# Attention and MLP in one kernel: in the first batch the softmax division moves from the probabilities to the output of head pairs

## The chip, the cores and the metric

The kernel runs on one core of one Trainium2 chip. The metric is the device time in microseconds (us) of one execution; every time here is in us unless marked ns. The engines are TensorE (PE in the rows; its weight loads are PEld), VectorE (DVE), ScalarE (ACT), GpSimd (POOL) and SyncE (SP), which issues the DMAs. Each works through its own list of instructions in order, and semaphores make one wait for another.

## What is computed

Three layers in fp32, on 4 batches of 576 tokens with 8 heads of 64:

```python
scores = (q @ k.T) / 8 + (cum_i - cum_j)      # decay; masked above the diagonal
attn = exp(scores - max(scores))
attn = attn / (sum(attn) + 1e-9)              # the division that the change moves
x = attn @ v                                  # per head; heads side by side: 2304 x 512
h = x @ w_in                                  # 512 x 2048
x2 = (h * sigmoid(1.702 * h)) @ w_out         # 2048 x 512
# then a soft mixture of 8 experts over 32 slots, on x2: 2304 x 512 out
```

## The kernel before

**Precision.** Matmul operands are split into a high and a low part (`kh` and `kl`, `pth` and `ptl`, `xh` and `xl`, and so on): ScalarE or VectorE makes the high part by a copy that rounds, VectorE or GpSimd the low part by a subtraction.

**Stages.** `run` (line 374) gives every engine the same sequence of batches. In batch 0 (`begin`) attention runs alone: the MLP has no input yet. From then on the MLP of batch b is laid between the attention steps of batch b + 1, in units. At the end come the last MLP alone and the expert layer.

**Slots.** `batch_steps` (line 88) writes each engine's order out by hand, in slots. Slot s holds the scoring of head s (scores, decay, Exp, sums) and the second half of head s - 1 (transposes of its probabilities, PV, output). The first batch has slots 0 to 8; slot 0 has no second half, and slot 8 scores head 0 of batch 1, while its second half is head 7 of batch 0. What the order lists of the first batch are (lines 148, 150 and 153) can be read in the code below. The steps that the text speaks of:

- `qk` of the head after next's slot: six transposes of q and k on TensorE into bank `xb` (line 924), then ScalarE makes `qs` (587) and `kh` (589), VectorE the low part of q (711) and `kl` (715). `dup`: GpSimd doubles `kh` and `kl` into the other 64 partitions (534, 536), by adding a column of zeros from `mask`, repeated.
- `score` in four groups g = 0 to 3: matmuls into `yb` (944, 946). The query rows of a head stand in five tiles, 0 to 4; group 0 is tile 4 (64 rows, 576 columns), then tile 3 (512), tiles 2 and 0 (384, 128), and tile 1 (256). VectorE adds the decay and takes the minimum (728), ScalarE takes Exp with the sum (595). Group 0 of the next head comes early, at the end of a slot (`early`).
- `vsplit` (VectorE 735, GpSimd 542), then `norm`: VectorE adds 1e-9 to the sums (740), takes the reciprocal (742) into `rsum`, and scales tiles 0 to 3 of `prob` in place (747); ScalarE scales tile 4 (602).
- `pt` in four chunks c = 0 to 3: TensorE transposes the scaled tiles into `zb` (963); ScalarE copies to `pth` (608), VectorE subtracts to `ptl` (753).
- `fill`: 16 matmuls into `mb`, the MLP's banks, whose results nobody reads (969; only in the first batch).
- `pv_first` and `pv`: TensorE multiplies v by `pth` and `ptl` into `xb` (990), with the part of v's high half in partitions 0 to 63 and of its low half in 64 to 127. `pv_first` also waits for `kl` of a later head, because `xb` holds q and k's transposes too. ScalarE copies the lower half to `olow` (613), and VectorE adds both halves into `xst` (759), 64 partitions for an even head and 64 for an odd one, so that a pair of heads fills one tile of `xst`.
- `xsplit`, in slot 8: ScalarE makes `xh` (617), VectorE `xl` (764) from the four tiles of `xst`; TensorE's MLP (1041) starts behind them.
- `weights` and `split`: in a few slots a 128x512 piece of the MLP's weights is loaded and split, by VectorE (705) and GpSimd (571).

Semaphores: `expd` counts Exp tiles, `sum_inv` reciprocals, `normed` and `normed_4` the scalings, `o_sum` the output sums.

Of the kernel before, what the change touches and what calls it, by code (L numbers as in the profile page):

```python
# [28 lines left out]
P = 128  # L29
# [17 lines left out]
S4_AT = 224  # L47
TURNS = [[(0, 0, 0), (0, 1, 0), (0, 2, 0), (0, 3, 0)],
# [39 lines left out]
def batch_steps(engine, begin, heads, following, mlp):  # L88
# [13 lines left out]
    for slot in range(0 if begin else 1, HEADS + 1):  # L102
# [9 lines left out]
        def at(yes, *step):  # L112
            return [(ahead, step)] if yes else []
# [16 lines left out]
        norm = at(scoring, "norm", s)  # L130
        end = at(scoring, "vsplit", s) + norm
        pv_first, pv = at(before, "pv_first", s - 1), at(before, "pv", s - 1)

# [8 lines left out]
        if begin:  # L142

            steps += [(0, ("weights", t)) for t in {1: (0, 1), 4: (2,), 5: (3,), 6: (4,), 7: (5,)}.get(slot, ())]
            steps += [(0, ("split", slot - 3))] if 2 < slot < 7 else []

            if engine == "pe":
                steps += pt(0) + pt(1) + score(1) + score(2) + qk + pt(2) + score(3) + pt(3) + at(before, "fill", s - 1) + pv_first + early + pv
            elif engine == "act":
                steps += (pt(0) + score(0) + pt(1) + score(1) + qk + pt(2) + score(2) + dup + pt(3) + score(3)  # L150
                          + norm + early_x + pv + xs[3])
            else:
                steps += (pt(0) + score(1) + pt(1) + score(2) + qk + pt(2) + score(3) + dup + pt(3)
                          + end + early + early_x + pv + xs[3])
            continue
# [15 lines left out]
def build(nc, q, k, v, f, w_in, w_out, phi, w1, w2, out):  # L171
    ctx = ExitStack()
    with ctx:
# [70 lines left out]
        rsum = sb("rsum", [P, 2, QT], F32, att_mem)  # L244
# [47 lines left out]

        xbf = xb[:, :, :].rearrange("p a n -> p (a n)")
# [38 lines left out]
        normed_4 = sem("normed_4")  # L332
        p_tr = sem("p_tr")
# [180 lines left out]
        def _(pool):  # L514
# [12 lines left out]
            def step(b, m, st):  # L527
# [10 lines left out]
                elif st[0] == "vsplit":  # L538
# [4 lines left out]
                                       vs[:, s % 2, :, 0:DIM].bitcast(F32), ALU.subtract).then_inc(v_split, 1)  # L543
                elif st[0] == "split":
# [34 lines left out]
        def _(act):  # L579
# [3 lines left out]
            def step(b, m, st):  # L583
# [6 lines left out]
                elif st[0] == "score":  # L590
                    s, par = st[1], st[1] % 2
                    for i in SCORE_ORDER[st[2]]:
                        w, r = P * i + QW[i], QW[i]
                        act.wait_ge(decayed, b * 40 + 5 * s + TILE_RANK[i] + 1)
                        nc.scalar.activation(prob[0:r, par, POFF[i]:POFF[i] + w], prob[0:r, par, POFF[i]:POFF[i] + w],  # L595
                                             ACT.Exp, bias=m_row[0:r, par, i:i + 1], scale=-1.0,
                                             accum_out=sums[0:r, par, i:i + 1]).then_inc(expd, 1)
                elif st[0] == "norm":
# [3 lines left out]
                    nc.scalar.activation(t, t, ACT.Copy, scale=rsum[0:QW[4], par, 4:5]).then_inc(normed_4, 1)  # L602
# [11 lines left out]
                elif st[0] == "xsplit":  # L614
                    kt = st[1]
                    act.wait_ge(o_sum, m * 8 + 2 * kt + 2)
# [63 lines left out]
        def _(dve):  # L680
# [26 lines left out]
            def step(b, m, st):  # L707
# [28 lines left out]
                elif st[0] == "norm":  # L736
# [5 lines left out]
                    nc.vector.reciprocal(rsum[:, par, :], sums_e[:, par, :]).then_inc(sum_inv, 1)  # L742
                    dve.wait_ge(sum_inv, n + 1)
                    for i in range(QT - 1):
                        w, r = P * i + QW[i], QW[i]
                        t = prob[0:r, par, POFF[i]:POFF[i] + w]
                        ins = nc.vector.tensor_scalar(t, t, rsum[0:r, par, i:i + 1], None, ALU.mult)  # L747
# [7 lines left out]
                elif st[0] == "pv":  # L755
# [4 lines left out]
                                            olow[r0:r0 + 64, :], ALU.add).then_inc(o_sum, 1)  # L760
                elif st[0] == "xsplit":
# [147 lines left out]
        def _(pe):  # L909
# [5 lines left out]
            def step(b, m, st):  # L915
# [241 lines left out]
```

## Time and profile before

| | |
|---|---|
| median of 3 runs | 823.66 us (822.15 to 827.57) |
| profiled execution | 823.54 us, of which the span in the trace 821.7 |
| busy, share of the span | PE 91%, PEld 85%, DVE 65%, ACT 46%, POOL 46% |
| first batch alone (attention without MLP) | about 9 to 107 us |
| chain of waits over the whole span, by engine | PE 64%, DVE 16%, issue 8%, ACT 4%, DMA 4% |

A share of busy time is an average over stages. The first batch, about an eighth of the span, is the only stretch in which the changed steps run, and there the engines stand otherwise than over the whole: it has to be read by itself. "Idle before" with an arrow names what ended a wait.

### The profile page before, as it was taken

Reading aid. Unit: us, or ns where it says so; the run is one execution under the profiler, and the core shown is the slowest. Engines: PE = TensorE matmul, PEld = TensorE weight load, DVE = VectorE, ACT = ScalarE, POOL = GpSimd, SP = SyncE. Lnnn points to the kernel's source line nnn. Section 1 sums busy time; section 2 is a strip of 40 time slices with the busy share of each in tenths; the row PEclk is TensorE's granted clock in tenths of the full one; section 3 lists DMA queues with packets and bytes.
Section 4 is the critical chain, followed back from the end, with each engine's and each line's share of the span. In section 5 each row is a group of like instructions: output and inputs, shape, how many; then the busy total and the mean of one; then the engine's idle time right before and its main releaser. Section 6 shows DMA issues by size and latency. Waiting matters only on the chain.

```text
span 821.7 us, 16948 instructions
## 1 busy us (share of the span) xinstructions
PE 751.1 (91%) x5993; PEld 698.9 (85%) x5993; DVE 534.7 (65%) x1430; ACT 374.5 (46%) x903; POOL 376.8 (46%) x394
## 2 busy tenths in 40 slices
PE   3899978999999699999999989999998999996996
PEld 2788878998999689999999889999998999993552
DVE  5899966777677676777777577777675444434323
ACT  3677754545454554546364454545443222111113
POOL 2344335565655165656474164747460776620000
PEclk9999989999999999999999699999999999997995
DMA  4433313333333113333334013333320545497976
GB/s 97 99 85 103 98 33 86 90 90 84 89 98 107 39 53 82 88 95 88 88 88 117 17 45 88 88 89 93 96 65 26 167 148 194 136 346 277 402 307 230
DMA packets 96518, 96.77 MB, mean 118 GB/s; under 512 B 61296, under 2 KB 61296, under 8 KB 96432
## 3 DMA queue, kind: packets, MB, share of 16 engines
q1 hardware_dynamic: 96432, 95.66, 38.5%
q8 instruction: 50, 0.82, 0.4%
q14 instruction: 36, 0.29, 0.1%
HBM read 90.84 MB, written 4.79 MB: 116 GB/s over the span
## 4 chain that ended last, share of the span: by engine, by line
PE 64%; DVE 16%; issue 8%; ACT 4%; DMA 4%; POOL 2%; SPq 1%; DVEq 0%; ACTq 0%; POOLq 0%
PE mb L1041 43%; PE yb L944 4%; PE zb L963 4%; PE xb L990 4%; DVE prob L747 3%; DMA qk_in<-in_k 2%; DVE ptl L753 2%; DMA ring_b<-in_moe_w 2%; PE mb L1016 2%; DVE qs L711 2%; ACT prob L595 1%; DVE kl L715 1%; PE xb L924 1%; PE mb L1080 1%; PE zb L1136 1%
## 5 line engine op out<-in xcount | busy, mean ns | idle before, releaser
L1041 PE MATMUL mb<-xh,wih 128*128 128x288 f32 x512 | 163.5, 319 | 11.4 <-DVE hid L813 7.0
L1041 PE MATMUL mb<-gh,woh 128*128 128x288 f32 x512 | 157.5, 308 | 3.8 <-DVE hid L813 3.8
L1041 PE MATMUL mb<-xl,wih 128*128 128x288 f32 x512 | 155.3, 303 | 0.0
L1041 PE MATMUL mb<-xh,wil 128*128 128x288 f32 x512 | 155.0, 303 | 0.0
L1041 PE MATMUL mb<-gl,woh 128*128 128x288 f32 x512 | 151.0, 295 | 0.0
L1041 PE MATMUL mb<-gh,wol 128*128 128x288 f32 x512 | 151.0, 295 | 0.0
L554 POOL TENSOR_TENSOR gl<-hid,gh 128x288 fp32r<-128x288 f32 x128 | 113.1, 890 | 57.1 <-ACT gh L636 55.8
L571 POOL TENSOR_TENSOR wol<-stage,woh 128x512 fp32r<-128x512 f32 x64 | 82.5, 1288 | 120.0 <-DVE woh L705 120.0
L813 DVE SCALAR_TENSOR_TENSOR hid<-gate,mb 128x288 f32<-128x288 f32 x128 | 57.6, 452 | 103.4 <-ACT gate L642 101.8
L595 ACT ACTIVATE prob<-prob,m_row 64x576 f32<-64x576 f32 (+4 forms) x160 | 96.4, 604 | 59.4 <-DVE m_row L728 58.8
L571 POOL TENSOR_TENSOR wil<-stage,wih 128x512 fp32r<-128x512 f32 x64 | 82.6, 1291 | 81.9 <-DVE wih L705 81.9
L1041 PEld LDWEIGHTS mb<-xh,wih 128*128 128x128 f32 x512 | 100.5, 196 | 13.2 <-DVE hid L813 8.1
L642 ACT ACTIVATE gate<-mb 128x288 f32<-128x288 f32 x128 | 52.7, 411 | 110.6 <-PE mb L1041 110.0
L608 ACT CAST pth<-zb 128x512 fp32r<-128x512 f32 (+1 forms) x128 | 62.9, 492 | 87.5 <-PE zb L963 83.7
L1041 PEld LDWEIGHTS mb<-xl,wih 128*128 128x128 f32 x512 | 100.8, 197 | 0.0
L1041 PEld LDWEIGHTS mb<-xh,wil 128*128 128x128 f32 x512 | 100.5, 196 | 0.0
L1041 PEld LDWEIGHTS mb<-gh,woh 128*128 128x128 f32 x512 | 96.7, 189 | 4.4 <-issue 2.8
L1041 PEld LDWEIGHTS mb<-gl,woh 128*128 128x128 f32 x512 | 96.6, 189 | 0.0
L1041 PEld LDWEIGHTS mb<-gh,wol 128*128 128x128 f32 x512 | 96.3, 188 | 0.0
L728 DVE CUSTOM_DVE_ANT_0 prob<-yb,cum_b 64x576 f32<-64x576 f32 (+4 forms) x160 | 83.5, 537 | 3.2 <-issue 3.0
L963 PE MATMUL zb<-ident,prob 128*128 128x128 f32 x480 | 76.1, 283 | 7.1 <-DVE prob L747 4.4
L753 DVE TENSOR_TENSOR ptl<-zb,pth 128x512 fp32r<-128x512 f32 (+1 forms) x128 | 72.9, 569 | 14.5 <-ACT pth L608 14.2
(145 smaller groups left out, 1450.3 us busy)
## 6 DMA issues: line engine op xcount, KB each, us to landing
stage<-in_moe_w_in SPq DMA_DIRECT2D x64, 256.0 KB, 3.3
stage<-in_moe_w_out SPq DMA_DIRECT2D x64, 256.0 KB, 2.7
ring_a<-in_moe_w SPq DMA_DIRECT2D x16, 1024.0 KB, 7.5
ring_b<-in_moe_w SPq DMA_DIRECT2D x14, 1024.0 KB, 11.6
cum_b<-cum_dram SPq DMA_DIRECT2D x32, 288.0 KB, 4.1
qk_in<-in_q SPq DMA_DIRECT2D x32, 144.0 KB, 3.3
qk_in<-in_k SPq DMA_DIRECT2D x32, 144.0 KB, 3.7
v_in<-in_v SPq DMA_DIRECT2D x32, 128.0 KB, 3.3
```

The source lines that it names most:

```text
L554: pool.tensor_tensor(gl[:, i % FT, HALF * (i // FT):HALF * (i // FT + 1)], hid[:, i % RING, :], gh[:, i % FT, HALF * (i // FT):HALF * (i / ...
L571: pool.tensor_tensor(lo[:, t, :], stage[:, t % 2, :], hi[:, t, :].bitcast(F32), ALU.subtract).then_inc(w_lo, 1)
L595: nc.scalar.activation(prob[0:r, par, POFF[i]:POFF[i] + w], prob[0:r, par, POFF[i]:POFF[i] + w], ACT.Exp, bias=m_row[0:r, par, i:i + 1], s ...
L608: nc.scalar.copy(pth[:, lo:hi], zb[:, c % 2, 0:hi - lo]).then_inc(p_hi, 1)
L642: nc.scalar.activation(gate[:, j % RING, :], mb[:, u % 2, 0:HALF], ACT.Tanh, scale=GATE / 2).then_inc(h_tanh, 1)
L728: nc.vector.tensor_tensor_reduce(prob[0:r, par, o:o + w], ybf[0:r, base:base + w], cum_b[0:r, par, 0:w], 1.0, 3e38, ALU.add, ALU.min, m_ro ...
L753: nc.vector.tensor_tensor(ptl[:, lo:hi], zb[:, c % 2, 0:hi - lo], pth[:, lo:hi].bitcast(F32), ALU.subtract).then_inc(p_lo, 1)
L813: nc.vector.scalar_tensor_tensor(out=hid[:, j % RING, :], in0=gate[:, j % RING, :], scalar=1.0, in1=bank[:, 0:HALF], op0=ALU.add, op1=ALU. ...
L944: mm(ybf[0:r, base + k0:base + k0 + kw], qs[:, par, P * i:P * i + r], x[:, par, k0:k0 + kw], start=not last, stop=last, skip_group_check=True)
L963: ins = tr(zb[:, c % 2, at:at + P], prob[:, par, POFF[i] + P * kt:POFF[i] + P * kt + P], swapped if back else ident)
L990: ins = mm(pv_ps[:, lo:q1], vs[:, par, kt, :], x[:, at:at + q1 - lo], start=(kt == 0 and x is pth), stop=(kt == (1 if q1 == 256 else 4) an ...
L1041: ins = mm(bank[:, 0:HALF], a[:, t, P * (j % 4):P * (j % 4) + P], x[:, t, cols], start=(i == 0), stop=(i == 11))
```

## The change

In the first batch, for heads 0 to 7, the probabilities are no longer scaled. `norm` becomes `sums`, which ends with the reciprocals; TensorE's transposes wait for the last Exp (`expd`) in place of the scaling. From batch 1 on `norm` is as before. In place of the scalings, for each pair of heads:

- `widen`, GpSimd, once a head, behind `vsplit`: writes each row's reciprocal 64 times side by side into `wide` (5 query tiles x 2 heads x 64), by adding the repeated zero column of `mask`. `wide` lies in `x2t`, which the MLP doesn't use yet.
- `spread`, TensorE, once a pair, in the even slots 2, 4, 6 and 8, between `pt` 1 and the first score group: five transposes of `wide` into the MLP's banks `mb`, so that each of the 128 rows of a pair's output finds its factors along the columns. ScalarE copies the 128x576 result to `spread_sb`, behind Exp of the first score group and ahead of the `qk` copies. `fill` waits for that copy.
- `scale`, VectorE, once a pair, right behind the output sum of the odd head: `xst` times `spread_sb`, 128x576. `xsplit` on ScalarE waits for it in the first batch.

`rsum` gets four rows in place of two.

```diff
@@ batch_steps
+        late_norm = begin and slot < HEADS
+        norm = at(scoring, "sums" if late_norm else "norm", s)
         end = at(scoring, "vsplit", s) + norm
+        if engine == "pool" and late_norm:
+            end = end + at(True, "widen", s)
+        spread = at(begin and before and s % 2 == 0, "spread", s - 1)
         pv_first, pv = at(before, "pv_first", s - 1), at(before, "pv", s - 1)
+        if engine == "dve":
+            pv = pv + at(begin and before and s % 2 == 0, "scale", s - 1)
...
             if engine == "pe":
-                steps += pt(0) + pt(1) + score(1) + score(2) + qk + pt(2) + score(3) + pt(3) + at(before, "fill", s - 1) + pv_first + early + pv
+                steps += pt(0) + pt(1) + spread + score(1) + score(2) + qk + pt(2) + score(3) + pt(3) + at(before, "fill", s - 1) + pv_first + early + pv
             elif engine == "act":
-                steps += (pt(0) + score(0) + pt(1) + score(1) + qk + pt(2) + score(2) + dup + pt(3) + score(3)
+                steps += (pt(0) + score(0) + pt(1) + score(1) + spread + qk + pt(2) + score(2) + dup + pt(3) + score(3)
                           + norm + early_x + pv + xs[3])
@@ GpSimd
+                elif st[0] == "widen":
+                    s = st[1]
+                    pool.wait_ge(sum_inv, s + 1)
+                    wait_from(pool, spread_tr, s // 2)
+                    pool.tensor_tensor(wide[:, :, s % 2, :], rsum[:, s % 4, :].unsqueeze(2).broadcast_to([P, QT, DIM]),
+                                       mask[:, 0:1].unsqueeze(1).broadcast_to([P, QT, DIM]), ALU.add).then_inc(widened, 1)
@@ ScalarE
+                elif st[0] == "spread":
+                    pair = (b * 8 + st[1]) // 2
+                    act.wait_ge(spread_tr, pair + 1)
+                    wait_from(act, x_scaled, pair)
+                    nc.scalar.copy(spread_sb, spread_ps).then_inc(spread_out, 1)
...
                 elif st[0] == "xsplit":
                     kt = st[1]
-                    act.wait_ge(o_sum, m * 8 + 2 * kt + 2)
+                    if isinstance(m, int) and m == 0:
+                        act.wait_ge(x_scaled, kt + 1)
+                    else:
+                        act.wait_ge(o_sum, m * 8 + 2 * kt + 2)
@@ VectorE
-                    nc.vector.reciprocal(rsum[:, par, :], sums_e[:, par, :]).then_inc(sum_inv, 1)
+                    nc.vector.reciprocal(rsum[:, s % 4, :], sums_e[:, par, :]).then_inc(sum_inv, 1)
+                    if st[0] == "sums":
+                        return
...
+                elif st[0] == "scale":
+                    n = b * 8 + st[1]
+                    kt = n // 2
+                    dve.wait_ge(spread_out, kt + 1)
+                    dve.wait_ge(o_sum, n + 1)
+                    nc.vector.tensor_tensor(xst[:, kt, :], xst[:, kt, :], spread_sb, ALU.mult).then_inc(x_scaled, 1)
@@ TensorE
-                    if c == 0:
-                        pe.wait_ge(normed, b * 8 + s + 1)
-                    if c == 1:
-                        pe.wait_ge(normed_4, b * 8 + s + 1)
+                    n = b * 8 + s
+                    if isinstance(n, int) and n < HEADS:
+                        if c == 0:
+                            pe.wait_ge(expd, 5 * n + 5)
+                    elif c == 0:
+                        pe.wait_ge(normed, n + 1 - HEADS)
+                    elif c == 1:
+                        pe.wait_ge(normed_4, n + 1 - HEADS)
...
+                elif st[0] == "spread":
+                    n = b * 8 + st[1]
+                    pe.wait_ge(widened, n + 1)
+                    wait_from(pe, spread_out, n // 2)
+                    for i in range(QT):
+                        ins = tr(spread_ps[:, P * i:P * i + QW[i]], wide[0:QW[i], i, :, :].rearrange("p h d -> p (h d)"),
+                                 ident[0:QW[i], 0:QW[i]])
+                    ins.then_inc(spread_tr, 1)
                 elif st[0] == "fill":
+                    wait_from(pe, spread_out, (b * 8 + st[1] + 1) // 2)
```

## Rows read from the trace of the kernel before

**Rows 1.** Busy by stretch: length, PE, PEld, DVE, ACT, POOL, granted clock, DMA, GB/s.
```profile
40.00:60.00 20.00, 18.64 (x144) 16.62 (x144) 19.13 (x60) 15.62 (x38) 9.45 (x11) 1.00 0.38 88
```

**Rows 2.** Chain of waits, first batch: start, duration, engine, tile, line.
```profile
35.88 0.67 DVE xst L759
...
93.82 0.67 DVE xst L759
```

**Rows 3.** Timeline of one period, VectorE: start, duration, engine, line, operation, shapes, count.
```profile
62.18 0.19 DVE L742 RECIPROCAL rsum<-sums_e 128x5 f32<-128x5 f32 x1
...
62.41 1.54 DVE L747 TENSOR_SCALAR prob<-prob,rsum 128x128 f32<-128x128 f32 x4
...
63.87 0.74 DVE L728 CUSTOM_DVE_ANT_0 prob<-yb,cum_b 64x576 f32<-64x576 f32 x1
...
64.65 0.75 DVE L759 TENSOR_TENSOR xst<-xb,olow 64x576 f32<-64x576 f32 x1
...
65.43 0.43 DVE L705 CAST wih<-stage 128x512 fp32r<-128x512 f32 x1
...
65.78 0.69 DVE L753 TENSOR_TENSOR ptl<-zb,pth 128x512 fp32r<-128x512 f32 x1
...
66.39 0.69 DVE L728 CUSTOM_DVE_ANT_0 prob<-yb,cum_b 128x512 f32<-128x512 f32 x1
...
67.00 0.69 DVE L753 TENSOR_TENSOR ptl<-zb,pth 128x512 fp32r<-128x512 f32 x1
...
68.50 0.75 DVE L711 SCALAR_TENSOR_TENSOR qs<-xb,qs 64x576 fp32r<-64x576 f32 x1
...
69.28 0.76 DVE L715 TENSOR_TENSOR kl<-xb,kh 64x576 fp32r<-64x576 f32 x1
```

**Rows 4.** Timeline of the same period: GpSimd, TensorE and ScalarE.
```profile
61.98 0.89 POOL L542 TENSOR_TENSOR vs<-v_in,vs 128x320 fp32r<-128x320 f32 x1 [0.27 <-DVE vs L735]
...
63.27 0.28 PE L990 MATMUL xb<-ptl,vs 128*128 128x64 f32 x1
...
63.58 0.64 ACT L613 COPY olow<-xb 64x576 f32<-64x576 f32 x1 [0.40 <-PE xb L990]
...
63.99 0.97 PEld L963 LDWEIGHTS zb<-ident,prob 128*128 128x128 f32 x9 [0.56 <-DVE prob L747]
...
67.11 0.72 ACT L595 ACTIVATE prob<-prob,m_row 128x512 f32<-128x512 f32 x1 [0.60 <-DVE m_row L728]
...
67.83 0.63 ACT L587 ACTIVATE qs<-xb 64x576 fp32r<-64x576 f32 x1
...
68.24 1.98 PE L969 MATMUL mb<-mask_r,ident_r 128*128 128x128 f32 x16
...
70.29 0.36 PE L990 MATMUL xb<-pth,vs 128*128 128x256 f32 x1
...
70.37 1.15 POOL L536 TENSOR_TENSOR kl<-kl,mask 64x576 fp32r<-64x576 f32 x1
...
71.62 0.32 PE L944 MATMUL yb<-kh,qs 128*64 128x288 f32 x1
```

**Rows 5.** Timeline, end of slot 0: VectorE and TensorE.
```profile
22.57 1.73 DVE L747 TENSOR_SCALAR prob<-prob,rsum 128x128 f32<-128x128 f32 x4
...
23.50 0.31 PE L946 MATMUL yb<-mask_r,ident_r 64*64 64x64 f32 x1
...
24.35 0.90 PE L963 MATMUL zb<-ident,prob 128*128 128x128 f32 x3 [0.54 <-DVE prob L747]
```

**Rows 6.** Timeline at the first batch's end, then (last row) busy time by stretch.
```profile
103.10 2.08 DVE L764 TENSOR_TENSOR xl<-xst,xh 128x576 fp32r<-128x576 f32 x3
...
105.21 0.75 DVE L759 TENSOR_TENSOR xst<-xb,olow 64x576 f32<-64x576 f32 x1
...
107.59 0.60 PE L1041 MATMUL mb<-xh,wih 128*128 128x288 f32 x1 [4.31 <-DVE xl L764]
...
107.00:111.00 4.00, 3.41 (x14) 3.40 (x15) 0.45 (x1) 1.08 (x4) 0.00 (x0) 0.50 0.00 0
```

More of the change, by code:

```diff
@@ L47 @@
 S4_AT = 224
+SPREAD_AT = 128
 TURNS = [[(0, 0, 0), (0, 1, 0), (0, 2, 0), (0, 3, 0)],
@@ L129, in batch_steps @@
             qk, dup = qk + dup, []
-        norm = at(scoring, "norm", s)
+        late_norm = begin and slot < HEADS
+        norm = at(scoring, "sums" if late_norm else "norm", s)
         end = at(scoring, "vsplit", s) + norm
+        if engine == "pool" and late_norm:
+            end = end + at(True, "widen", s)
+        spread = at(begin and before and s % 2 == 0, "spread", s - 1)
         pv_first, pv = at(before, "pv_first", s - 1), at(before, "pv", s - 1)
+        if engine == "dve":
+            pv = pv + at(begin and before and s % 2 == 0, "scale", s - 1)
         xs = [at(s == 0 and before, "xsplit", t) for t in range(KM)]
@@ L243, in build @@
         sums_e = sb("sums_e", [P, 2, QT], F32, att_mem)
-        rsum = sb("rsum", [P, 2, QT], F32, att_mem)
+        rsum = sb("rsum", [P, 4, QT], F32, att_mem)
         f_sb = prob[0:BATCH * HEADS, 0, 0:SEQ]
@@ L291, in build @@
         zb = pb("zb")
+        x2_flat = x2t[:, :, :].rearrange("p t n -> p (t n)")
+        wide = x2_flat[:, 0:QT * 2 * DIM].rearrange("p (i h d) -> p i h d", i=QT, h=2)
+        spread_sb = x2t[:, 2, :]
+        spread_ps = mb[:, :, :].rearrange("p a n -> p (a n)")[:, SPREAD_AT:SPREAD_AT + SEQ]
         xbf = xb[:, :, :].rearrange("p a n -> p (a n)")
@@ L332, in build @@
         normed_4 = sem("normed_4")
+        widened = sem("widened")
+        spread_tr = sem("spread_tr")
+        spread_out = sem("spread_out")
+        x_scaled = sem("x_scaled")
         p_tr = sem("p_tr")
@@ L601, in step @@
                     t = prob[0:QW[4], par, POFF[4]:POFF[4] + SEQ]
-                    nc.scalar.activation(t, t, ACT.Copy, scale=rsum[0:QW[4], par, 4:5]).then_inc(normed_4, 1)
+                    nc.scalar.activation(t, t, ACT.Copy, scale=rsum[0:QW[4], st[1] % 4, 4:5]).then_inc(normed_4, 1)
                 elif st[0] == "pt":
@@ L735, in step @@
                     nc.vector.tensor_copy(vs[:, s % 2, :, 0:DIM], v_in[:, s % 2, :, :]).then_inc(v_hi, 1)
-                elif st[0] == "norm":
+                elif st[0] in ("sums", "norm"):
                     s, par = st[1], st[1] % 2
@@ L746, in step @@
                         t = prob[0:r, par, POFF[i]:POFF[i] + w]
-                        ins = nc.vector.tensor_scalar(t, t, rsum[0:r, par, i:i + 1], None, ALU.mult)
+                        ins = nc.vector.tensor_scalar(t, t, rsum[0:r, s % 4, i:i + 1], None, ALU.mult)
                     ins.then_inc(normed, 1)
```

## The prediction

> **What bounds the kernel now.** The change touches only the first batch, so I first asked the busy table by stretch what bounds that part. In [rows 1] VectorE is busy 19.13 of 20 us, TensorE 18.64, ScalarE 15.62, GpSimd 9.45, at a granted clock of 1.00. VectorE looks like the bound, and the change takes work from it. But a busy share doesn't say what the freed time is worth: the next wait does. So I took the chain of waits, where the first batch shows one pattern per head. The sum of a head's output ends its PV product and stands in it at 35.88 for head 0 and at 93.82 for head 6 [rows 2]: six periods, (93.82 - 35.88) / 6 = 9.66 us each. Then the timeline of one period, VectorE first [rows 3], the other engines second [rows 4].
>
> The four scalings of `prob` by `rsum` stand at 62.41 and take 1.54 us; VectorE gets on with the next tile at 63.87, so their slot in its queue is 63.87 - 62.41 = 1.46 us [rows 3]. Behind them wait the decay of tile 4 of the next head (63.87), then the output sum `xst` (64.65), then the next head's first `ptl` (65.78 behind a weight cast). On TensorE the last matmul of PV starts at 63.27 and lasts 0.28; ScalarE copies the low half to `olow` from 63.58 to 64.22 [rows 4]. The sum needs that copy. So it starts at 64.65 now and can't start before about 64.25, whatever VectorE has to do. What is late next after the scalings is PV, only 0.40 us behind them.
>
> And PV hangs on VectorE's own later work. After `xst` come `ptl`, decay, `ptl` (67.00 to 67.69), then TensorE's third score group and the 16 fill matmuls (68.24 to 70.22), and then PV at 70.29; beside it VectorE makes `kl` by 70.04, which PV awaits too [rows 3, 4]. This closes a loop: PV, `olow`, `xst`, `ptl`, decay, `ptl`, score, fill, PV. One turn costs one period, 9.66 us; of it only 0.40 us is the scaling. The reader is to see that VectorE is full, yet the loop runs through it only in part, and that anything put into the loop is paid in full.
>
> **The change part by part.**
>
> (a) *Scalings removed, heads 0 to 7.* 1.46 us of VectorE's queue each, 11.7 us in all, but worth 0.40 us where the loop closes behind it. That is so at the end of the first batch's slots 1 to 7: 7 x 0.40 = 2.8 us gained. ScalarE's scaling of tile 4 (0.78 us, between the last Exp and `olow`) goes as well; ScalarE waits for PV behind it, so nothing. TensorE's first transposes wait for the last Exp in place of the scaling: they start at 63.99, behind an idle time that ends with the scaling [rows 4], and could start at some 63.55, but their product is next used by VectorE behind `xst`, so nothing more.
>
> (b) *Slot 0* has no PV. There the transposes of head 0 wait for the scaling alone: TensorE's early score ends at about 23.65 (last matmul at 23.50) and the transposes start at 24.35 [rows 5]. Gain 0.7 us; bounds 0.54 (the idle time that the row shows) and 0.85.
>
> (c) *The scale of a head pair on VectorE*, 4 times: 128x576, two SBUF inputs. The same form is `xl`: three take 2.08 us, 0.69 each [rows 6]. It also waits for the sum before it, which costs the overlap of some 0.08 that neighbours in the queue have (66.39 + 0.69 ends after the next starts at 67.00 [rows 3]). I take 0.75 us (bounds 0.61 and 0.78). It stands right behind `xst` and ahead of the next `ptl`, in the loop, with nothing beside it that hides it: 4 x 0.75 = 3.0 us lost. The last of them delays the cast of the fourth x tile, which in the seam starts as soon as `xst` is done (105.21 + 0.75, then the cast, `xl`, and TensorE's first MLP matmul at 107.59 [rows 6]).
>
> (d) *The copy of the spread out of PSUM on ScalarE*, 4 times, slots 2, 4, 6 and 8, placed ahead of the q copy. Its price: `olow` (64x576 from PSUM) is 0.64 us [rows 4]; no 128x576 copy from PSUM is in the trace, and columns set the time of the others, so 0.64. In the row, Exp runs 67.11 to 67.83, the q copy 67.83 to 68.46, and VectorE's q step starts at 68.50 [rows 3, 4]: ScalarE goes ahead without a gap and VectorE waits for it. So the q step moves from 68.50 to 69.14 and `kl` ends at 70.68 in place of 70.04. PV then starts after 70.75 in place of 70.29, a delay of about 0.5. But GpSimd's doubling of `kl` starts at 70.37 and lasts 1.15, and TensorE's early score comes right after it at 71.62 [rows 4]; it moves by the whole 0.64. I take 0.62 (bounds: 0.24, if only TensorE's fill, which now also waits for this copy, counted; 0.76, with VectorE's small gap ahead of the q step added). 4 x 0.62 = 2.5 us lost.
>
> (e) *TensorE's spread*, five transposes a pair: nine take 0.97 us to issue [rows 4], so 0.11 each, 0.55 us. It stands ahead of the first score group. That group can begin 0.44 us earlier than now (a), so it comes 0.1 us later; the decay that reads it starts 0.6 us after its `ptl` and still finds it done. Nothing. Its cover is the time from PV's end to that decay; if it goes, 0.55 x 4 = 2.2 us.
>
> (f) *GpSimd's widening*, eight times, 128x640 in halves of 320 columns. The nearest row is the v split, 320 columns, 0.89 us [rows 4]. It comes behind that split (61.98 to 62.87) and behind the reciprocal (62.18 + 0.19 [rows 3]), so it ends at about 63.8; TensorE wants it at about 64.5, after the nine transposes. Next in GpSimd's queue are a weight split, which waits for VectorE until after `xst`, and the doublings of `kh`, behind the copies that follow 67.83, and of `kl` at 70.37: all far off. Nothing, with 0.7 us in hand.
>
> (g) `rsum` with four rows, and the counts of `normed` less 8 from batch 1 on: no time. DMA issues and SyncE's order don't change. Batches 1 to 3 have the same instructions and move as a block.
>
> **Sum.** -0.7 - 2.8 + 3.0 + 2.5 = +2.0 us. The profiled execution took 823.54 us (span 821.7 and 1.84 around it), so 825.5; it lies 0.12 below the median of the three runs, 823.66, so the comparison holds for the median too.
>
> **A rule weighed.** The scalings in [rows 3] take 1.54 us with GpSimd's v split beside their start, 61.98 to 62.87 [rows 4]; VectorE's tensor-tensor operations don't show such a neighbour's cost in these rows. By the terms above the scale of a pair, at about 65, and the widening, until 63.8, don't meet. The Trainium skill ("SBUF — State Buffer", Who interferes with whom) says that a VectorE instruction with two SBUF inputs contends with a GpSimd instruction that reads SBUF, and the later one waits for the whole of the other; the new scale is such an instruction and speaks against this change. By it the sum would be that of the collision below, if the two met.
>
> **The rivals.**
>
> *VectorE stays the bound.* If the work freed were all worth its time: 8 x 1.46 - 4 x 0.75 = 8.7 us gained, 814.8. For it: 19.13 of 20 busy. Against it: `olow` ends 0.4 us ahead of `xst`, in a fixed order. Chance 0.04.
>
> *The copy is hidden.* If ScalarE or the queue behind it had more room than I read, (d) is nothing: 825.5 - 2.5 = 823.0. For it: ScalarE is idle 4.4 of 20 us. Against it: not there. Chance 0.15.
>
> *The seam costs more.* Between PV of head 7 and the first MLP matmul at 107.59 TensorE has little to do, and in the stretch behind it its granted clock is 0.50, the 1.2 GHz level [rows 6]. The gap grows by 0.75 us. If the low level lasts longer for it, up to the whole of that 4 us stretch at half rate again, 2 to 3 us come on top: about 828. Chance 0.13.
>
> *Collision.* Each pair's scale waits for a widening of 0.89: 4 x 0.89 = 3.6, 829.1. Against it: the 1.2 us between them. Chance 0.04.
>
> *The widening is late: slower by more.* Place: TensorE's spread, ahead of the first score group, with the whole queue (scores, q and k transposes, fill, PV) behind it. It decides once a widening takes over 0.89 + 0.7 = 1.6 us; from there each us costs four. With both operands repeated by a stride of zero, it is unlike the row; at four times its 0.89, 3.6 us, it would be 4 x 2.0 = 8.0, together 833.5. For it: no row has this form. Against it: the doubling of k in [rows 4] also adds a repeated zero column, 576 columns in 1.15. Chance 0.06.
>
> That the change does nothing isn't a case: the scalings are gone from the code.
>
> **How the numbers follow.** The forecast, the loop with (c) and (d) paid, has 0.58. Its bounds are 823.4 (0.24 for the copy and 0.61 for the scale) and 826.2. The runs scatter from 822.15 to 827.57. From the hidden copy less that scatter, to the collision, 821.5 to 829.5 leaves out the first rival and the last, one in ten. 1% is 8.2 us, about what a measurement tells from no change: only the first rival is faster by that (0.04), only the last slower (0.06 with its upper part, 0.05 taken), the rest is within: 0.91.
>
> **What would show it.** In the profile after: `xst` waits for `olow`, VectorE idle some 0.8 us ahead of it in the first batch; VectorE's share there below 19 of 20; periods of alternating length, about 9.9 and 10.0 with a copy or a scale, against 9.66; no idle time of TensorE behind the widening; the first MLP matmul near 109.6 in place of 107.59. The forecast is wrong if that matmul comes before 107 or after 112, or if times move behind it by more than the shift.

## The result: slower, by about 1%

| | median of the executions | the profiled one | span |
|---|---|---|---|
| before | 824.62 us (822.15 to 827.57, 4) | 823.54 us | 821.7 |
| changed | 833.68 us (827.54 to 837.80, 4) | 827.54 us | 825.7 |

Ratio 1.0135, 95% interval 1.0081 to 1.019. The predicted 825.5 (821.5 to 829.5) is too low. The changed kernel was timed twice more beside the experiments: 1.0077 (1.0048 to 1.0106) and 1.0164 (1.0102 to 1.0225). The ratios leave out executions over 1.5% above their kernel's fastest, and in the set of the third (1.0164) that takes 7 of 23 off the kernel before; over all executions of that set it is 1.0118. Over all executions whose span is on record (75 before, 20 changed) the mean span is 821.3 and 829.8: 8.6 us, with a standard error of 0.9. Single executions of the kernel before scatter over some 20 us, those of the changed one over 12, so the profiled one of the changed kernel, the fastest of its four, shows only 4.0 of them.

**The first batch after the change.** The busy table, for [rows 1]:

```profile
40.00:60.00 20.00, 18.57 (x142) 16.48 (x142) 16.35 (x52) 13.88 (x36) 10.26 (x12) 1.00 0.35 88
```

VectorE's share fell from 19.13 to 16.35 of 20 us, and TensorE did no more than before (18.57 against 18.64). Work was taken away and nothing got faster. (L numbers are those of the changed kernel.) The timeline at the end of slot 4, for [rows 3, 4]:

```profile
63.09 0.19 DVE L771 RECIPROCAL rsum<-sums_e 128x5 f32<-128x5 f32 x1
...
63.64 0.74 DVE L757 CUSTOM_DVE_ANT_0 prob<-yb,cum_b 64x576 f32<-64x576 f32 x1 [0.36 <-issue]
...
63.74 0.71 POOL L563 TENSOR_TENSOR x2t<-rsum,mask 128x320 f32<-128x320 f32 x1
...
64.49 0.63 ACT L639 COPY olow<-xb 64x576 f32<-64x576 f32 x1 [1.64 <-PE xb L1040]
...
65.16 0.75 DVE L790 TENSOR_TENSOR xst<-xb,olow 64x576 f32<-64x576 f32 x1 [0.76 <-ACT olow L639]
...
66.01 0.76 DVE L797 TENSOR_TENSOR xst<-xst,x2t 128x576 f32<-128x576 f32 x1
...
66.69 0.42 DVE L734 CAST wih<-stage 128x512 fp32r<-128x512 f32 x1
```

The output sum waits 0.76 us for `olow`, ScalarE waits 1.64 for PV ahead of that, and the scale (0.76) stands between the sum and everything behind it. The widening takes 0.71, behind the v split. Slot 2, VectorE and ScalarE:

```profile
36.88 0.69 DVE L757 CUSTOM_DVE_ANT_0 prob<-yb,cum_b 128x512 f32<-128x512 f32 x1 [0.39 <-issue]
...
39.52 0.75 DVE L740 SCALAR_TENSOR_TENSOR qs<-xb,qs 64x576 fp32r<-64x576 f32 x1 [0.65 <-ACT qs L608]
```

```profile
37.60 0.73 ACT L616 ACTIVATE prob<-prob,m_row 128x512 f32<-128x512 f32 x1 [0.66 <-DVE m_row L757]
...
38.33 0.62 ACT L623 COPY x2t<-mb 128x576 f32<-128x576 f32 x1
38.84 0.64 ACT L608 ACTIVATE qs<-xb 64x576 fp32r<-64x576 f32 x1
```

ScalarE's copy (0.62) comes between Exp and the q copy, and VectorE's q step waits 0.65 for it. Besides, the decay of the 512-column tile waits 0.39 us for its scores, with TensorE's five transposes ahead of them. The same stretch before, then after (last matmul of PV, last matmul of the scores, decay; the decay after is the first row above):

```profile
34.53 0.28 PE L990 MATMUL xb<-ptl,vs 128*128 128x64 f32 x1
...
36.76 0.22 PE L946 MATMUL yb<-mask_r,ident_r 128*128 128x128 f32 x1
...
37.19 0.69 DVE L728 CUSTOM_DVE_ANT_0 prob<-yb,cum_b 128x512 f32<-128x512 f32 x1
```

```profile
34.16 0.28 PE L1040 MATMUL xb<-ptl,vs 128*128 128x64 f32 x1
...
35.31 0.80 PE L1013 MATMUL mb<-ident,x2t 128*128 128x128 f32 x5
...
36.61 0.23 PE L983 MATMUL yb<-mask_r,ident_r 128*128 128x128 f32 x1
```

Counted from PV's last matmul, the scores come 36.76 - 34.53 = 2.23 us behind it before and 36.61 - 34.16 = 2.45 after, so 0.22 later. VectorE is ready for the decay 2.66 us behind it before and 36.88 - 0.39 - 34.16 = 2.33 after, so 0.33 earlier, since the scalings no longer hold it up. The two together used up the slack. The end of the batch, for [rows 6], TensorE, and the clock behind it:

```profile
110.80 0.60 PE L1091 MATMUL mb<-xh,wih 128*128 128x288 f32 x1 [5.17 <-DVE xl L801]
```

```profile
107.00:111.00 4.00, 0.20 (x1) 0.21 (x2) 2.79 (x4) 1.77 (x3) 0.00 (x0) 0.50 0.00 0
111.00:115.00 4.00, 4.00 (x18) 3.98 (x19) 0.39 (x2) 0.66 (x3) 0.00 (x0) 0.50 0.00 0
115.00:119.00 4.00, 4.00 (x24) 3.92 (x24) 1.85 (x7) 1.32 (x3) 1.76 (x2) 0.75 0.21 66
```

The first MLP matmul starts at 110.80, 3.2 us later than before, and TensorE waits 5.17 us ahead of it (4.31 before). The 3.2 us are those of the two profiled executions; over all that were traced they are 2.5 (below).

### The profile page after: what moved, and what is told of

It is laid out like the page before. It is cut to its first block, busy times and chain, and to the rows that moved or that the text cites. A ratio compares the mean times of both kernels' runs of the same rounds, so it can differ in the third digit from the quotient of the medians.

```text
span 825.7 us, 16989 instructions
## 1 busy us (share of the span) xinstructions
PE 753.2 (91%) x6013; PEld 700.6 (85%) x6013; DVE 525.5 (64%) x1402; ACT 369.9 (45%) x899; POOL 381.5 (46%) x402
## 4 chain that ended last, share of the span: by engine, by line
PE 68%; DVE 14%; issue 7%; DMA 5%; ACT 3%; POOL 2%; SPq 1%; DVEq 0%; ACTq 0%; POOLq 0%
PE mb L1091 42%; PE xb L1040 6%; PE yb L981 5%; PE zb L1004 4%; DMA qk_in<-in_k 3%; PE mb L1066 2%; DMA ring_b<-in_moe_w 2%; DVE prob L778 2%; DVE woh L734 1%; PE xb L961 1%; DVE ptl L784 1%; PE yb L983 1%; POOL wol L592 1%; PE zb L1186 1%; PE mb L1130 1%
## 5 line engine op out<-in xcount | busy, mean ns | idle before, releaser
L1091 PE MATMUL mb<-xh,wih 128*128 128x288 f32 x512 | 161.0, 314 | 12.2 <-DVE hid L850 7.1
L1091 PE MATMUL mb<-xl,wih 128*128 128x288 f32 x512 | 153.0, 299 | 0.0
L1091 PE MATMUL mb<-xh,wil 128*128 128x288 f32 x512 | 152.8, 298 | 0.0
L1091 PEld LDWEIGHTS mb<-xh,wih 128*128 128x128 f32 x512 | 98.3, 192 | 13.6 <-DVE hid L850 7.6
L1091 PEld LDWEIGHTS mb<-xl,wih 128*128 128x128 f32 x512 | 98.4, 192 | 0.0
L1091 PEld LDWEIGHTS mb<-xh,wil 128*128 128x128 f32 x512 | 98.2, 192 | 0.0
```

The lines of the kernel that those rows point to most:

```text
L1091: ins = mm(bank[:, 0:HALF], a[:, t, P * (j % 4):P * (j % 4) + P], x[:, t, cols], start=(i == 0), stop=(i == 11))
```

## The experiments

Three readings are used. *Seven periods*: from VectorE's q step in slot 1 to that in slot 8 of the first batch (before: 29.95 to 97.23, 67.28 us). It repeats within 0.15 us, since the start of slot 1 is left out: it varied by 1 us between executions of one kernel, with the moment at which TensorE's clock rose for good in the first batch (28.2, 28.1 and 25.6 us in the three of the changed kernel). *Near 250 us*: the q step of head 16, batch 2's first (before: 247.84, in a second execution 249.35). *The whole*: the ratio of timed executions.

| kernel | seven periods | first MLP matmul | near 250 us | ratio, 95% interval | mean clock |
|---|---|---|---|---|---|
| before | 67.28, 67.27 | 107.59, 108.30 | 247.84, 249.35 | 1 | 0.957 |
| changed | 69.99, 70.00, 70.03 | 110.80, 110.76, 109.79 | 251.40, 251.69, 250.35 | 1.008 to 1.016, three times | 0.953 |
| drop_all | 64.47 | 103.89 | 245.64 | one execution, 823.51 us | 0.957 |
| late_spread | 66.63, 66.77 | 106.97, 107.08 | 246.83, 247.29 | 1.0019 (0.9978 to 1.006) | 0.955 |
| late_scale | 68.69, 68.63 | 109.38, 109.67 | 253.51, 249.53 | 1.0102 (1.0036 to 1.0167) | 0.949 |
| moved | 64.62 | 105.49 | 245.29 | 0.9987 (0.9951 to 1.0024) | 0.956 |
| shift_start | 67.30 | 111.33 | 252.31 | 1.005 (1.0023 to 1.0077) | 0.956 |
| shift_seam | 67.29 | 111.67 | 249.21 | 1.0063 (1.0029 to 1.0098) | 0.953 |
| before_warm | 67.32 | 108.35 | 246.73 | 1.0052 (1.0018 to 1.0085) | 0.958 |
| after_warm | 70.05 | 110.48 | 247.75 | 1.0103 (1.0054 to 1.0151) | 0.956 |
| moved_warm | 64.51 | 104.79 | 243.36 | 1.0038 (0.9998 to 1.0077) | 0.957 |
| before_hold | 67.28 | 108.32 | 248.79 | 1.0159 (1.0082 to 1.0235) | 0.950 |
| moved_hold | 64.44 | 105.05 | 247.41 | 1.0144 (1.0076 to 1.0211) | 0.953 |

**What the removal alone is worth: drop_all.** The edit, in the changed kernel:

```diff
-            end = end + at(True, "widen", s)
-        spread = at(begin and before and s % 2 == 0, "spread", s - 1)
+        spread = []
-            pv = pv + at(begin and before and s % 2 == 0, "scale", s - 1)
```

> The changed kernel without widening, spread and scale: the first batch's attention output is not divided by its row sums at all. It leaves only what the removal of the scalings is worth. Loop theory: 0.40 us for each of slots 1 to 7 and some 0.4 for slot 0, so the first MLP matmul at 107.59 - 3.2 = 104.4. Rival, that VectorE is the bound and its freed time counts in full: 8 x 1.46 = 11.7 earlier, 96.

Seven periods took 64.47, so 2.81 us less than before, 0.40 for each: the loop theory to the digit, and VectorE as the bound is out. The first MLP matmul, at 103.89, came half a us ahead of the 104.4 expected; slot 0 made the difference. In this kernel too the sum waits for `olow`:

```profile
71.67 0.75 DVE L785 TENSOR_TENSOR xst<-xb,olow 64x576 f32<-64x576 f32 x1 [0.76 <-ACT olow L637]
```

**Both additions out of the loop: moved.** TensorE's five transposes go behind the fill, which has five matmuls fewer there; ScalarE's copy goes behind the last Exp, where it waits for PV anyway; VectorE scales pairs 0 to 2 a slot later, ahead of the sum, where it waits for `olow`.

```diff
-            pv = pv + at(begin and before and s % 2 == 0, "scale", s - 1)
+            pv = at(begin and slot in (3, 5, 7), "scale", s - 2) + pv + at(begin and slot == HEADS, "scale", s - 1)
...
-pt(0) + pt(1) + spread + score(1) ... + at(before, "fill", s - 1) + pv_first
+pt(0) + pt(1) + score(1) ... + at(before, "fill", s - 1) + spread + pv_first
...
-pt(1) + score(1) + spread + qk ... + pt(3) + score(3)
+pt(1) + score(1) + qk ... + pt(3) + score(3) + spread
```

> The changed kernel with its two additions taken out of the loop: ScalarE copies the spread after the last Exp of the slot, where it waits for PV, TensorE turns it right behind the fill (which has 5 matmuls fewer in those slots, so TensorE's work is the same), and VectorE scales pairs 0 to 2 one slot later, ahead of the output sum, where it waits for olow. Its outputs are right. Loop theory (mine): slots 1 to 7 gain 0.40 us each and slot 0 some 0.4, the last scale costs 0.8: the first MLP matmul 2.4 us earlier than before, at about 105.2, and the time 822 if the rest moves as a block. Rival, that VectorE's freed time is worth more once these are out: earlier than 104. Rival, that the transposes or the copy still cost: 107 or later.

Seven periods: 64.62, within 0.15 us of the kernel that does nothing in place of the scalings. What was moved is hidden but for that, and the first MLP matmul comes 2.1 us earlier than before. In this execution the sum still waits for `olow` in a slot without a scale:

```profile
62.88 0.75 DVE L790 TENSOR_TENSOR xst<-xb,olow 64x576 f32<-64x576 f32 x1 [0.76 <-ACT olow L639]
```

The whole, though, is undecided: 0.9987, the interval on both sides of 1.

**One at a time: late_spread and late_scale.** late_spread has the second and third of the three edits above (and the shorter fill), late_scale the first; each was profiled once and then timed.

> The changed kernel with only the spread moved: TensorE's five transposes right behind the fill, which has 5 matmuls fewer in those slots, and ScalarE's copy behind the last Exp of the slot. The scales stay behind the output sum of the odd head. Its outputs are right. Loop theory, from the difference of the changed kernel (110.80) and the kernel with both moved (105.49), 5.3 us, less 2.4 for the scales: 2.9 us for the four spreads, first MLP matmul at 107.9. Rival, that the scale costs all 5.3: 110.8.

> The changed kernel with only the scale moved: pairs 0 to 2 are scaled one slot later, ahead of the output sum, where VectorE waits for olow; the last pair as in the changed kernel. The spread stays where the change put it. Its outputs are right. Read by when the first MLP matmul starts (before 107.59, changed 110.80, twice within 0.04 in two executions). Loop theory: three scales of some 0.8 leave the loop, 108.4. Rival, that the scale is hidden anyway and the spread costs all: 110.8.

With the scale alone in the loop (late_spread), seven periods cost 66.63 - 64.47 = 2.16 us and 2.30 more than drop_all, for the three scales that fall within them: 0.72 to 0.77 each. With the spread alone (late_scale) they cost 68.69 - 64.47 = 4.22, for four spreads: 1.05 each. My expectation had them at 2.4 and 2.9, from the sum of both. The spread's price in late_scale isn't its price in the changed kernel, and late_scale's timeline shows why. Slot 4, GpSimd, VectorE, TensorE, VectorE:

```profile
52.98 1.90 POOL L563 TENSOR_TENSOR x2t<-rsum,mask 128x320 f32<-128x320 f32 x1
...
53.55 0.74 DVE L797 TENSOR_TENSOR xst<-xst,x2t 128x576 f32<-128x576 f32 x1
...
54.93 0.86 PE L1013 MATMUL mb<-ident,x2t 128*128 128x128 f32 x5 [0.22 <-POOL x2t L563]
...
56.55 0.68 DVE L757 CUSTOM_DVE_ANT_0 prob<-yb,cum_b 128x512 f32<-128x512 f32 x1 [0.48 <-issue]
```

Slot 8 of the same execution, where the scale starts as the widening ends:

```profile
92.22 0.71 POOL L563 TENSOR_TENSOR x2t<-rsum,mask 128x320 f32<-128x320 f32 x1
...
92.93 0.74 DVE L797 TENSOR_TENSOR xst<-xst,x2t 128x576 f32<-128x576 f32 x1
```

The scale's new place puts it beside the widening of slots 4 and 6, and there the widening takes 1.90 us in place of 0.71. So it is in all five traces with the scale moved: the ten widenings that overlap a scale take 1.90 or 1.91, the other 78 of all traces 0.71 or 0.72. TensorE's spread then waits for it, starts 0.55 us behind `xst` in place of 0.17 in the changed kernel, and holds up the scores. That makes the decay wait in all four slots with a spread (0.38, 0.48, 0.49 and 0.40 us), and 4 x 0.62 + 1.75 = 4.23, for the 4.22 measured. In the changed kernel the widening meets no scale; the decay waits only in slots 2 and 8 (0.39 and 0.40), since in slots 4 and 6 a weight cast (0.41 at 55.89) holds up VectorE by as much. There the two additions cost 3 x 0.75 + 4 x 0.62 + 0.79 = 5.5, for 69.99 - 64.47 = 5.52. So about 1 us of late_scale's 4.22 is this collision, which the edit itself brought in, and the spread's own price in its old place is 3.3 us, 0.8 each. In moved the widening is as long, but the spread stands late enough not to wait for it.

> The kernel with only the spread moved out of the loop, now timed: its first MLP matmul came 0.6 us earlier than before in one execution. Block theory: as the kernel before, less some 0.6 us, ratio 0.999. Own-cost theory (something of the changed first batch, whichever part, is paid again in the later batches, 3 to 6 us): ratio 1.003 or more. If the spread in its old place is what is paid again: 0.999, and the kernel with only the scale moved high.

> The kernel with only the scale moved out of the loop, timed: its first MLP matmul came 1.8 us after that of the kernel before in one execution. Block theory: ratio 1.002. If the spread in its old place is what is paid again in the later batches: 1.006 or more. If the scale was: 1.002.

Timed, the kernel with the scale in the loop can't be told from the kernel before (1.0019), and the one with the spread in it is slower (1.0102). Over all executions of this set they stand 0.6 and 7.3 us above the kernel before (standard errors 1.6 and 1.9). So the spread's old place is the costly part, in the first batch as in the whole; up to 1 us of the 7.3 is the collision.

**Does the rest move as a block: shift_start and shift_seam.** In the kernel before, two memsets of VectorE (1.98 and 1.02 us; what follows comes 3.55 later), ahead of the scan of log f, respectively ahead of the output sum of head 7.

```diff
+            nc.vector.memset(x2t[:, :, :], 0.0)
+            nc.vector.memset(hid[:, :, :], 0.0)
```

> The kernel before with two more memsets of together about 3 us on VectorE ahead of the cumulated log f, so that everything from the first head on starts some 3 us later, in its old order and with its old gaps. Its outputs are right. Block theory: 824.6 + 3 = 827.6. Phase theory, if what matters is the absolute time at which the MLP begins: as the changed kernel, 832 or more, with a wide spread. If what matters is the pattern of the first batch or the changed code, not the time: 827.6.

> The kernel before with the same two memsets (about 3 us) in VectorE's queue right ahead of the output sum of head 7, so that only the gap between the last PV of batch 0 and the first MLP matmul grows, from 5.5 to about 8.5 us. Block theory: 827.6. Seam theory (the longer gap costs clock behind it): 828 to 831, with a longer stretch at 0.50 after the first MLP matmul. Phase theory: 832 or more, as shift_start.

A shift at the start is paid once: ratio 1.005, some 4.1 us for the 3.55, with an interval from 1.9 to 6.3. So the time at which the MLP begins doesn't by itself cost anything that this resolves. With the wider gap ahead of the MLP, the first MLP matmul came 3.7 us late and the mark near 250 us only 0.6 (both against the means of the two executions before, 107.95 and 248.6), and the whole cost 5.2 us. The seam theory's number fits (828.66), its mechanism doesn't: between the first MLP matmul and the mark near 250 TensorE was at the low level for 3.0 us in this trace, against 9.4 and 10.7 before, so the low level did not last longer behind the wider gap. (One execution of shift_seam took 3249 us; it is left out of all means.)

**Where executions of one kernel part: before_look, after_again, after_third.** No edit.

> The kernel before, unaltered, for a second profiled execution. Clock theory (the executions of one kernel part at the batch boundaries, by how long TensorE's clock stays at 0.50 there, and the first batch is the same in all): the first MLP matmul at 107.6 within 0.1, the same times to within 0.5 up to 250 us, and behind that other stretches at 0.50 than in the first execution and an end that differs by 1 to 6 us. Rival, that the changed kernel's extra time behind 250 us is its own: the second execution follows the first to within 1 us to the end, 821 to 823 us of span.

> The changed kernel once more, unaltered, to see how its executions spread. In the profiled execution the first MLP matmul comes 3.2 us later than before and the end 4.0 us later, but the other three executions took 6 to 10 us more. Block theory (the later batches only move along; the high runs were chance): most executions near 828, median 827 to 829. Phase theory (the later batches react to when they begin, by stalls or a low clock that some executions have and others not): a wide spread again, 827 to 838, median 832 to 834.

> The changed kernel a third time, for its size. Up to 250 us two of its executions run 3.6 us behind the kernel before, within 0.3 of one another; behind that they part, by as much as 6 us, with the length of the stretches in which TensorE's clock is granted at 0.50. Block theory with scatter: the ratio comes near 1 + 3.6 / 824 = 1.0044, in an interval that reaches below 1.005. Own-cost theory (the change costs more than its shift, in the later batches): 1.007 to 1.009 again, interval above 1.005.

before_look ended at 824.5 (span), 2.8 us behind the first; but it was 0.7 us late at the first MLP matmul already and 1.5 near 250, where the clock theory wanted 0.1 and 0.5. after_again (median 830.3) fell between both theories, and after_third's ratio is above both. The three executions of the changed kernel stand within 1.4 us near 250, and their spans end at 825.7, 831.9 and 826.3. TensorE's row for the boundary between the MLPs of batches 0 and 1 (busy, granted clock, DMA, GB/s), for before, changed, and changed again:

```profile
240.00:320.00 80.00, 70.98 (x520) 0.94 0.28 74
```

```profile
240.00:320.00 80.00, 71.10 (x525) 0.94 0.26 69
```

```profile
240.00:320.00 80.00, 73.59 (x493) 0.84 0.25 69
```

The granted clock of this stretch is 0.94 in two and 0.84 in the third, of the same kernel as the second. Its time at the 1.2 GHz level is 2 x (1 - 0.84) x 80 = 26 us against 10. From 251.69 - 251.40 = 0.3 us the two executions drift to 5.2 apart by 320 us. Over 193 timed executions of all kernels, a fit with one slope and one offset per kernel gives 0.34 us (standard error 0.01) for each us at the low level, and leaves 1.7 us of scatter. The Trainium skill ("TensorE: Matmul & The Clock Gate", Part 1: The HAM clock gate) says that the moment of the clock's rise varies by about half a us from run to run; the trace agrees that it varies, and by more: 28.2, 28.1 and 25.6 us in the three executions of the changed kernel.

**Filling the gaps: before_warm, after_warm, moved_warm; before_hold, moved_hold.** The first three add 40 matmuls into the MLP's banks behind the last PV of slot 8 (in two of them behind a wait for the spread's last copy); the other two add 20 at the head of slot 1 of every batch from 1 on.

```diff
+                elif st[0] == "warm":
+                    for _ in range(40):
+                        mm(mb[:, 0, 0:P], ident_r[:, :], mask_r[:, :], start=True, stop=True)
...
+                elif st[0] == "hold":
+                    pe.wait_ge(logits_out, m * QT + 1)
+                    for _ in range(20):
+                        mm(mb[:, 0, 0:P], ident_r[:, :], mask_r[:, :], start=True, stop=True)
```

> The kernel before with 40 more fill matmuls (4.4 us at the full clock, results read by nobody) on TensorE behind the last PV of slot 8, in the gap ahead of the first MLP matmul. Clock theory: the gap of 5.5 us is what brings the 0.50 stretch behind 107; with it filled that stretch is gone or much shorter, the first MLP matmul stays at 107.6, the unit after it comes 1.5 to 3 us earlier, and the time falls by some 1 to 3 us, to 821 to 823. Rival (no gain: the low clock comes whatever the gap holds, or the fill delays the transposes behind it): 824 or more.

> The changed kernel with the same 40 fill matmuls in its gap before the MLP (first matmul at 110.80, 13.7 us at 0.50 from 100 to 148 us, against 10.2 before). Clock theory, that part of the change's cost lies in the longer gap: it gains more than the kernel before does from the same fill, 2 to 4 us, and comes to 827 or less; what is left against the kernel before with the fill is the first batch's 3.2 us. Rival, that the extra lies elsewhere: it gains no more than the kernel before with the fill, 829 or more.

> The kernel with spread and scale moved out of the loop, and the 40 fill matmuls in its gap as well: the version that the experiments point to. Loop and clock theories together: first MLP matmul at 105.5 and 1.5 to 3 us less behind it: 819 to 821, ratio 0.993 to 0.997. Rival, that the later batches give it back (the kernel with nothing but the scalings removed ended no earlier than the kernel before in one execution): 823 or more.

> The kernel before with 20 fill matmuls (2.2 us at the full clock) on TensorE at the head of slot 1 of every batch from 1 on, where it waits 2.7 us for the first scaled tiles (283.3 to 286.0 in batch 2's case). Clock theory: the stretches at 0.50 around 284, 310, and 460 get shorter, the mean granted clock rises above 0.9575 and the time falls by up to 3 us; its scatter falls too. Rival (the low clock there comes from waits ahead of that place, and the fill at half rate delays the transposes by up to 2 us a batch): 826 or more.

> The kernel with spread and scale moved out of the loop, with the same 20 fill matmuls at the head of slot 1 of every batch from 1 on: a candidate for the fastest. Clock theory: 2 to 3 us below the kernel with both moved (822.3), ratio 0.994 to 0.997. Rival as for the kernel before with this fill: no better than 822, or above it.

At the seam the fill does what it should. In all fifteen traces without it TensorE's clock falls between 102 and 111 us, for 3.4 to 10.2 us; in the three with it that stretch is missing. TensorE from 100 to 148 us, before_warm (3.4 us at the low level; the kernel before has 10.2 and 13.7 in two executions, the changed one 13.7, 13.7 and 10.2):

```profile
100.00:148.00 48.00, 44.44 (x330) 0.96 0.23 64
```

And near 250 us each is ahead of its parent, by 1.9 us (246.73 against 248.6), 3.4 us (247.75 against a mean of 251.15) and 1.9 us (243.36 against 245.29). But the whole keeps it only in the changed kernel, 828.1 against 830 to 834; before_warm (1.0052, median 824.69) and moved_warm (1.0038, 823.15) show no gain, as their rivals had it, and after_warm's 828.1 lies between the clock theory and its rival. Over all executions of this set before_warm is 2.0 us above the kernel before (standard error 1.2) and moved_warm 0.4 (1.4), so that they end above their parents isn't clear, that they don't gain the 2 us is likelier; where they were lost no run shows. The fill inside the batches costs outright, 1.0159 and 1.0144, as the rival had it: it stands in TensorE's queue ahead of the transposes, and it didn't even fill the wait that it was meant for. In before_hold's batch 2:

```profile
286.70 4.52 PE L970 MATMUL mb<-mask_r,ident_r 128*128 128x128 f32 x20 [1.60 <-issue]
291.02 1.07 PE L963 MATMUL zb<-ident,prob 128*128 128x128 f32 x4
```

The wait before it runs to 286.70, the fill takes 4.52 us at the low level (2.43 at the full clock, at 102.7), and the transposes start at 291.02, 5 us later than in the kernel before (286.01), in an execution that was 0.9 late near 250; the mean clock fell in both. This doesn't test the clock theory at the later boundaries, it only shows that this place is wrong for it.

## Why the prediction was wrong

Point by point, first what held. The loop held: 0.40 us a period for the scalings (2.81 measured, 2.8 forecast). The scale held: 0.72 to 0.77 each in the loop, and 0.86 at the seam (the last q step to the first MLP matmul 11.22 us, 10.36 before), for 0.75. The copy's delay held: VectorE's q step waits 0.65 where 0.64 was forecast.

In the changed kernel the widening (0.71 us) is never waited for, and the rival of a late widening didn't happen. Nor did that of a collision: the widening ends at 64.45 and the scale starts at 66.01. The collision itself is real, though, as late_scale shows, and it comes out otherwise than that rival had it: the scale keeps its 0.74 us, and the widening takes 1.2 us longer. The Trainium skill's rule of two SBUF inputs ("SBUF — State Buffer", Who interferes with whom) has the two contend, and the trace agrees; it has the later one wait, and here it is the one that started first, the widening, that lasts longer. VectorE as the bound didn't happen either.

Slot 0's gain was forecast at 0.7, bounds 0.54 and 0.85. Its q step in slot 1 stands at 29.95 to 30.69 (mean 30.5) in the five traces that have the scalings and no shift ahead of them, and at 28.54 to 29.83 (mean 29.3) in the twelve without scalings: some 1.2 us, of which the moment of the clock's rise makes an unknown part.

**A term was mis-sized: (e), TensorE's spread, "Nothing".** It was costed in the stretch of [rows 3, 4], where a weight cast of VectorE (65.43) delays the decay by some 0.35 us. Slots 2 and 8 have no such cast; there the decay waits 0.39 and 0.40 us. The scores come 0.22 us later behind PV, for 0.1 forecast, and the forecast left out that its own gain (a) brings VectorE to the decay 0.33 earlier. That is 0.8 us, and it closes the seven periods: -2.8 + 4 x 0.62 + 3 x 0.75 + 0.8 = 2.7, measured 2.71. With it the first batch cost 2.5 us by the means of the executions (first MLP matmul 107.95 before, 110.45 changed), near the forecast of 2.0.

**The step that failed** is in (g): "Batches 1 to 3 have the same instructions and move as a block." Of the 8.6 us only 2.5 are the shift that the first batch hands on; the other 6 arise behind it, in code that the change doesn't touch. The experiments show in which kernels the step fails (mean span against the kernel before, with its standard error, and the first MLP matmul against its mean of 107.95):

| kernel | mean span | first MLP matmul | rest |
|---|---|---|---|
| changed | +8.6 (0.9) | +2.5 | 6.1 |
| late_scale | +8.7 (1.6) | +1.6 | 7.1 |
| late_spread | +1.0 (1.1) | -0.9 | 1.9 |
| moved | -2.3 (1.1) | -2.5 | 0.2 |
| shift_start | +3.9 (0.9) | +3.4 | 0.5 |
| shift_seam | +5.2 (1.0) | +3.7 | 1.5 |

The rest is clear of the scatter only in the two kernels that have the spread in its old place. The scale in the loop, a shift at the start and a wider seam don't bring it by themselves: moved and late_spread have the changed kernel's seam (11.2 us from the last q step). With the seam filled the picture is another: after_warm has a rest of 2.1 (1.2), before_warm of 1.6 (0.9) and moved_warm, without the spread in its old place, of 3.5 (1.1). So it is shown that the later batches pay again, and that without fill they do so where the spread stands in its old place; why isn't shown, since none of its instructions runs in the later batches.

About 2.7 of the 8.6 go with TensorE's clock: the mean granted clock fell from 0.9572 to 0.9529 over the timed executions, 7 to 8 us more at the low level, at 0.34 each. At equal clock the changed kernel is 5.9 us (standard error 0.45) above the kernel before, late_scale 3.7 (0.7), late_spread -0.4 (0.5), moved -3.2 (0.5), shift_start 3.2 and shift_seam 2.4. Less their shifts that leaves 3.4 and 2.1 for the first two, and 0.5 or less for the other four. The traces don't place them: the three profiled executions of the changed kernel happen to lie only 3.4 us above the two of the kernel before at equal clock, 2.5 of it the shift. This stays open.

The rival nearest by its number was the seam's, at 828 and 0.13, but its mechanism, a low level that lasts longer behind the seam, isn't what the traces show: from the first MLP matmul to the mark near 250 it is 9.6, 9.5 and 8.0 us in the changed kernel, against 9.4 and 10.7 before. No rival of the prediction priced what happens at the later boundaries. And the range's upper end came from three executions, 822.15 to 827.57; more of them showed 814 to 834 for the kernel before. The direction was forecast rightly, and so was the first batch to within half a us, in part by luck: slot 0 gained some 0.4 us more than forecast and hid half of the 0.8 that (e) left out.

## What to carry to other kernels

Find the loop first, and ask of every added instruction whether it stands in it: 11.7 us of VectorE's work were worth 2.8 in the seven periods and about 1 in slot 0, while the 3.0 us of scales put back cost all of their 3.0 (2.16 for three in the loop, 0.86 for the last at the seam), and three scales and four spreads in places where their engines waited anyway cost 0.15. When an instruction is moved, look at what the other engines do beside its new place: late_scale took the scale out of the loop and put it beside a widening. Cost an edit in every slot in which it runs, not in one: the weight cast that hid the spread was missing in two of four. And where the executions of one kernel differ by 1%, price what is behind an edit from several of them, not from one trace.

## What the runs showed of the hardware

- Two executions of the same kernel, 0.3 us apart near 250 us, were 5.2 us apart at 320, by how long TensorE's clock stood at its low level between (granted clock 0.94 and 0.84 over 240 to 320).
- A us at the low clock goes with 0.34 us in this kernel, by the fit, and not with the 0.5 that work at half rate would lose. That TensorE waits for other engines in the other part is the likely reason, not a measured one.
- A tensor-tensor of VectorE with two SBUF inputs (0.74) beside a tensor-tensor of GpSimd on 128x320 made the latter take 1.90 us in place of 0.71, ten times out of ten, and was itself not slowed (0.74 to 0.75).
- Twenty fill matmuls took 4.52 us at the low level and 2.43 at the full one.
- A start that is 3.55 us late is 3.4 to 3.7 late at the first MLP matmul (111.33) and some 4.1 at the end (1.9 to 6.3): no cost of absolute time shows beyond the scatter.
- 40 fill matmuls in a 5.5 us gap brought the time at the low level from 100 to 148 us from 10.2 and 13.7 us to 3.4, and yet no time at the end (before_warm, 1.0052); in the changed kernel the same fill brought about 4 us.
